# Attention and two mixers on one core: two score products per head from the third tile on, with queries and keys moved by DMAs

## The reference, cut to what matters

```python
# q, k, v: [2, 8, 768, 64] float32; n_sink = 4, window = 128
scores = scale * np.matmul(q, k.transpose(0, 1, 3, 2))
keep = is_sink | in_window            # first 4 keys, and the 128 keys up to the query
scores = np.where(keep, scores, -1e9)
a = softmax(scores)
x = np.matmul(a, v)                   # [2, 768, 512] once the heads are joined
# first mixer:
h = x.transpose(0, 2, 1) @ U @ V      # over tokens, rank 32
u = x + h.transpose(0, 2, 1)
x = u + np.maximum(u @ w_ch1, 0) @ w_ch2
# second mixer: the same with a relu of its own over tokens and other sizes
```

## Time and profile before

| what | us |
|---|---|
| three runs: median (lowest to highest) | 630.93 (630.76 to 631.37) |
| the profiled execution | 631.34 |
| its span, first to last instruction | 629.4 |
| TensorE busy / weight loads busy | 615.7 / 556.5 |
| VectorE, ScalarE, GpSimd busy | 352.6, 324.9, 402.5 |

### The profile page before, as it was taken

How to read it: one execution, slowest core, us unless ns; L and a number is a source line. 1 busy time by engine, 2 the same in 40 slices (tenths; PEclk the granted TensorE clock), 3 DMA queues, 4 the chain that set the end, 5 groups by cost and what they waited for, 6 DMA issues and landing times.

```text
span 629.4 us, 10364 instructions
## 1 busy us (share of the span) xinstructions
PE 615.7 (98%) x3468; PEld 556.5 (88%) x3468; DVE 352.6 (56%) x755; ACT 324.9 (52%) x727; POOL 402.5 (64%) x425
## 2 busy tenths in 40 slices
PE   7899999999999999999999999999999999999997
PEld 6888889999999989999999888899998888999986
DVE  6776664554564646776657731495667227665411
ACT  4666666556545555654544444544453447454321
POOL 7676547978979775665665744567566536666352
PEclk9999999999999999999999999999999999999999
DMA  8482343553343425313223332432324343421152
GB/s 165 94 189 52 84 101 103 134 123 105 96 115 93 151 75 153 100 65 118 85 89 96 111 100 81 128 101 68 117 84 118 112 123 84 150 84 35 51 157 76
DMA packets 88467, 65.59 MB, mean 104 GB/s; under 512 B 43040, under 2 KB 72480, under 8 KB 88416
## 3 DMA queue, kind: packets, MB, share of 16 engines
q1 hardware_dynamic: 88416, 64.95, 37.5%
HBM read 61.52 MB, written 3.15 MB: 103 GB/s over the span
## 4 chain that ended last, share of the span: by engine, by line
PE 87%; DVE 4%; issue 2%; ACT 2%; POOL 2%; DMA 1%; DVEq 0%; SPq 0%; ACTq 0%; POOLq 0%
PE bank L1621 34%; PE bank L1371 23%; PE bank L1586 10%; PE bank L1447 4%; PE bank L1417 3%; PE bank L1550 3%; PE bank L1500 3%; PE bank L1427 2%; PE bank L1526 1%; PE bank L1394 1%; POOL w_lo L879 1%; DVE masked L1142 1%; PE bank L1481 1%; PE bank L1613 1%; ACT probs L898 1%
## 5 line engine op out<-in xcount | busy, mean ns | idle before, releaser
L879 POOL TENSOR_TENSOR w_lo<-w_raw,w_hi 128x512 fp32r<-128x512 f32 (+1 forms) x158 | 210.2, 1337 | 138.3 <-ACT w_hi L912 137.3
L912 ACT ACTIVATE w_hi<-w_raw 128x512 fp32r<-128x512 f32 (+1 forms) x158 | 96.6, 618 | 53.9 <-PE bank L1621 35.9
L1621 PE MATMUL bank<-w_hi,hid_hi 128*128 128x512 f32 x216 | 86.4, 400 | 0.0
L1621 PE MATMUL bank<-w_hi,hid_lo 128*128 128x512 f32 x216 | 85.1, 394 | 0.0
L1621 PE MATMUL bank<-w_lo,hid_hi 128*128 128x512 f32 x216 | 84.8, 393 | 0.0
L898 ACT ACTIVATE probs<-masked,neg_max 128x264 f32<-128x264 f32 x96 | 49.5, 516 | 65.3 <-DVE neg_max L1142 64.8
L1621 PE MATMUL bank<-w_hi,y_hid 128*128 128x512 f32 x216 | 71.1, 394 | 0.2
L1142 DVE CUSTOM_DVE_ANT_0 masked<-bank,masks 128x264 f32<-128x264 f32 x96 | 41.0, 429 | 31.0 <-PE bank L1417 27.6
L1447 PE MATMUL bank<-v_nat,probs_T 128*128 128x64 f32 x352 | 50.2, 261 | 0.8 <-DVE probs_T L1161 0.5
L1447 PEld LDWEIGHTS bank<-v_nat,probs_T 128*128 128x128 f32 x352 | 47.9, 190 | 2.2 <-ACT probs_T L960 0.8
L1621 PEld LDWEIGHTS bank<-w_hi,y_hid 128*128 128x128 f32 x216 | 40.6, 188 | 9.5 <-POOL w_lo L879 1.5
(11 more groups left out here) (177 smaller groups left out, 1501.1 us busy)
## 6 DMA issues: line engine op xcount, KB each, us to landing
w_raw<-in_moe_w_ch_dram SPq DMA_DIRECT2D x144, 256.0 KB, 2.7
w_raw<-in_moe_w_ch_dram SPq DMA_DIRECT2D x20, 512.0 KB, 3.5
q_nat<-in_q_dram SPq DMA_DIRECT2D x12, 256.0 KB, 3.3
k_nat<-in_k_dram SPq DMA_DIRECT2D x12, 256.0 KB, 4.0
v_nat<-in_v_dram SPq DMA_DIRECT2D x12, 256.0 KB, 3.7
out_dram<-o_stage SPq DMA_DIRECT2D x11, 256.0 KB, 3.3
w_raw<-in_moe_w_tok_dram SPq DMA_DIRECT2D x6, 256.0 KB, 2.7
w_raw<-in_moe_w_tok_dram SPq DMA_DIRECT2D x8, 192.0 KB, 2.3
```

What stands on the lines that cost most here:

```text
L879: nc.gpsimd.tensor_tensor(w_lo[:, split % NW, 0:n], w_raw[:, split % NR, 0:n], w_hi[:, split % NW, 0:n].bitcast(f32), ALU.subtract) \
L912: nc.scalar.activation(w_hi[:, split % NW, 0:n], w_raw[:, split % NR, 0:n], ACT.Copy) \
L1621: last = mm(m_tile(use)[:, :], stationary, w[:, slot, :], start=False, stop=(final and n == 2), skip_group_check=True)
```

## The change

The number of the first tile with two products goes from 6 to 2 (`TWO_PASSES_FROM`). For tiles 0 and 1, with three products, the high keys are in an array of their own, `k_one`, which lies where `uT_hi` will be. The copies into the other half are DMAs on SP's queue now, in all tiles from 2 on: two for the queries when `q_hi` is cast, two for the keys when `k_hi` is cast. When tile 1's keys are cast, 12 DMAs bring them and the sinks from `k_one` into `k_hi`, both halves. VectorE's and ScalarE's copies in tiles 6 to 11 are gone, but for the sinks at the second batch's start. TensorE waits at a tile's first score for these DMAs.

```diff
+    TWO_PASSES_FROM = 2
...
+        def high_keys(T):
+            return k_one if T < TWO_PASSES_FROM else k_hi
...
         def query_low(eng, wait, T):
-            if T >= NQ:
+            if T >= TWO_PASSES_FROM:
...
+            def move_queries(T):
+                sp.wait_ge(q_high, T + 1)
+                for e in range(2):
+                    rows, there = slice(e * D, (e + 1) * D), slice((1 - e) * D, (2 - e) * D)
+                    sp.dma_start(q_both[there, T % 2, :, e, :].bitcast(f32), q_hi[rows, T % 2, :, :].bitcast(f32)) \
+                      .then_inc(q_there[T % 2], 16)
+
+            def move_keys(T):
+                sp.wait_ge(k_high, T)
+                for e in range(2):
+                    rows, there = slice(e * D, (e + 1) * D), slice((1 - e) * D, (2 - e) * D)
+                    sp.dma_start(k_hi[there, :, e, T % 3, 0:P].bitcast(f32), k_hi[rows, :, e, T % 3, 0:P].bitcast(f32)) \
+                      .then_inc(k_there[T % 2], 16)
+
+            def move_first_keys(T):
+
+                slot = T % 3
+                sp.wait_ge(k_first_high, 2)
+                sp.wait_ge(k_high, T)
+                for e in range(2):
+                    rows = slice(e * D, (e + 1) * D)
+                    for there in (rows, slice((1 - e) * D, (2 - e) * D)):
+                        sp.dma_start(k_hi[there, :, e, slot, :].bitcast(f32), k_one[rows, :, e, slot, :].bitcast(f32)) \
+                          .then_inc(k_there[slot], 16)
+                        for other in ((slot + 1) % 3, (slot + 2) % 3):
+                            sp.dma_start(k_hi[there, :, e, other, P:BLK].bitcast(f32),
+                                         k_one[rows, :, e, slot, P:BLK].bitcast(f32)).then_inc(ksinks_there, 16)
...
-                elif s[0] == "ksplit" and s[1] >= NQ:
-                    T = s[1]
-                    act.wait_ge(k_copied, T + 1)
-                    act.wait_ge(scores_ready, H * (T - 1))
-                    for e in range(2):
-                        src = list(key_parts(k_hi, T))[e][0]
-                        last = nc.scalar.activation(k_hi[(1 - e) * D:(2 - e) * D, :, e, T % 3, 0:P], src, ACT.Copy)
-                    last.then_inc(k_moved, 1)
...
                     nc.vector.tensor_copy(q_hi[:, T % 2, :, :], q_full).then_inc(q_high, 1)
-                    if T >= NQ:
-                        for e in range(2):
-                            rows, there = slice(e * D, (e + 1) * D), slice((1 - e) * D, (2 - e) * D)
-                            moved = nc.vector.tensor_copy(q_both[there, T % 2, :, e, :], q_full[rows])
-                        moved.then_inc(q_moved, 1)
...
+                        if T == TWO_PASSES_FROM:
+                            pe.wait_ge(k_there[1], 64)
+                            pe.wait_ge(ksinks_there, 128)
+                        if T >= TWO_PASSES_FROM:
+                            pe.wait_ge(q_there[T % 2], 32 * (T // 2))
+                            pe.wait_ge(k_there[T % 2], 32 * (T // 2) + 64 * (T % 2))
...
-                    if T < NQ:
-                        passes = ((high, k_hi), (high, k_lo), (low, k_hi))
+                    if T < TWO_PASSES_FROM:
+                        passes = ((high, k_one), (high, k_lo), (low, k_one))
                     else:
                         passes = ((q_both[:, T % 2, h // 2, h % 2, :], k_hi), (high, k_lo))
```

More of the change, by code:

```diff
@@ L365, in attention_then_two_mixers @@
             k_lo = eb("k_lo", [P, PAIRS, 2, 3, BLK], f32r)
+            with ExitStack() as before_uT:
+                k_one = before_uT.enter_context(nc.sbuf_tensor("k_one", [P, PAIRS, 2, 3, BLK], f32r))
             uT_hi = eb("uT_hi", [P, KD, S], f32r)
@@ L426, in attention_then_two_mixers @@
         klo_zeroed = sem("klo_zeroed")
+        q_there = [sem(f"q_there{i}") for i in range(2)]
+        k_there = [sem(f"k_there{i}") for i in range(2)]
+        ksinks_there = sem("ksinks_there")
         x2_added = sem("x2_added")
@@ L442, in attention_then_two_mixers @@
         q_high = sem("q_high")
-        q_moved = sem("q_moved")
         k_moved = sem("k_moved")
@@ L537, in queries_split @@
         def queries_split(T):
-            return T + 1 if T < NQ else 2 * (T + 1) - NQ
+            return T + 1 if T < TWO_PASSES_FROM else 2 * (T + 1) - TWO_PASSES_FROM
         def query_low(eng, wait, T):
-            if T >= NQ:
+            if T >= TWO_PASSES_FROM:
                 for e in range(2):
@@ L554, in key_low @@
         def key_low(eng, wait, T, e):
-            low, high = list(key_parts(k_lo, T))[e], list(key_parts(k_hi, T))[e]
+            low, high = list(key_parts(k_lo, T))[e], list(key_parts(high_keys(T), T))[e]
             steps = ((3, 2), (1, 0)) if T == 0 else ((1, 0),)
@@ L749, in _ @@
                     loaded = NR
+                elif s[0] == "qsplit" and s[1] >= TWO_PASSES_FROM:
+                    move_queries(s[1])
+                elif s[0] == "ksplit" and s[1] >= TWO_PASSES_FROM - 1:
+                    if s[1] == TWO_PASSES_FROM - 1:
+                        move_first_keys(s[1])
+                    else:
+                        move_keys(s[1])
                 if s in chunk_at:
@@ L917, in _ @@
                     act.wait_ge(q_split, queries_split(T - 1))
-                    if T > NQ:
-                        act.wait_ge(q_moved, T - NQ)
                     act.wait_ge(tp_ready, tp_at[s] + 1)
@@ L934, in _ @@
                     act.wait_ge(k_copied, 1)
-                    for src, dst, sinks, sink_dst in key_parts(k_hi, 0):
+                    for src, dst, sinks, sink_dst in key_parts(k_one, 0):
                         nc.scalar.activation(sink_dst, sinks, ACT.Copy)
                         nc.scalar.activation(dst, src, ACT.Copy).then_inc(k_first_high, 1)
-                elif s[0] == "ksplit" and s[1] >= NQ:
-                    T = s[1]
-                    act.wait_ge(k_copied, T + 1)
-                    act.wait_ge(scores_ready, H * (T - 1))
-                    for e in range(2):
-                        src = list(key_parts(k_hi, T))[e][0]
-                        last = nc.scalar.activation(k_hi[(1 - e) * D:(2 - e) * D, :, e, T % 3, 0:P], src, ACT.Copy)
-                    last.then_inc(k_moved, 1)
                 elif s[0] == "ksinks":
@@ L1062, in _ @@
             for part in (slice(0, 3, 2), slice(1, 2)):
-                nc.vector.memset(k_hi[:, :, :, part, :].rearrange("p a b s k -> p (a b) s k").bitcast(f32), 0.0) \
+                nc.vector.memset(k_one[:, :, :, part, :].rearrange("p a b s k -> p (a b) s k").bitcast(f32), 0.0) \
                   .then_inc(khi_zeroed, 1)
@@ L1118, in _ @@
                         dve.wait_ge(scores_ready, H * (T - 1))
-                    for src, dst, _, _ in key_parts(k_hi, T):
+                    for src, dst, _, _ in key_parts(high_keys(T), T):
                         last = nc.vector.tensor_copy(dst, src)
@@ L1401, in _ @@
                         pe.wait_ge(q_split, queries_split(T))
-                        if T >= NQ:
-                            pe.wait_ge(q_moved, T - NQ + 1)
-                            pe.wait_ge(k_moved, T - NQ + 2)
+                        if T == TWO_PASSES_FROM:
[4 more added lines that the diff above has]
+                            pe.wait_ge(k_there[T % 2], 32 * (T // 2) + 64 * (T % 2))
+                        if T == NQ:
+                            pe.wait_ge(k_moved, 1)
                         pe.wait_ge(k_split, keys_split(T) - (2 if T == 0 else 0 if T == NQ else 1))
```

2 lines of the change are left out of this document (removed).

## The result

The changed kernel takes 640.92 us (median of 4, 639.47 to 641.55) beside 631.11 us of the kernel before (4 runs): ratio 1.0154, 95% interval 1.0142 to 1.0166. The forecast was 632.8 with a range up to 636.0. The sign was right, but the loss is 9.8 us where 1.9 was forecast. The profiled execution took 641.43 us, with a span of 639.7.

What follows compares the result with a forecast made beforehand. VectorE's key casts, held by GpSimd, were taken to bound the first batch, TensorE the stretch from 80 to 200 us. Lost products (3.84 us) go into waiting, held casts net +1.92, moves zero: 632.8 us, range 629.7 to 636.0.

Steps and rivals of the forecast that it cites:

- What bounds: First batch: the end of VectorE's key casts sets each mark; from 80 to 200 us TensorE alone sets the time.
- what a product is worth: Score products of tiles 2 to 5: 0.12 us of TensorE each, 32 lost, 3.84 us.
- The rival with TensorE as the bound: Whole kernel: TensorE sets the end and every lost product shows, 627.1 us; chance 0.14.
- The held casts: Tiles 1 to 4: two GpSimd low-query subtractions (the pair) add 1.40 us and hold VectorE's key casts; sum +1.92 us.
- marks: Starts of line 1481 (x_nat with U) in tiles 1 to 5; forecast at 26.46, 37.38, 49.12, 61.50, 72.19 us.
- Case (b): Tiles 3 and 4: casts ready during the first half-subtraction, one slips in after each half, ending 0.29 us after the pair.
- The rival of casts that stay together: Tiles 3 and 4: both casts run after the first half, 0.93 us earlier in each; 631.0 us; chance 0.24.
- One sign of being right: Marks of tiles 2 to 5: TensorE idles 1.5 us or more before each.
- Hidden, by 0.7 us: Tile 2's first score, wanted at 29.69 us: last key move lands at 29.0, so SP's added moves cost nothing.
- The rival of late moves: Tile 2's last key move lands at 31.7 us, 2.0 late: 634.8 us; later tiles too, 636 and more; chance 0.15.
- the later tiles: First scores after tile 2: key moves land 3.1 us after the casts, wanted 4.39 after; hidden by 1.3 us.

Runs made afterwards that it cites:

- the run with both edits: Kernel before with low queries of tiles 2 to 5 as two GpSimd instructions and their third score product dropped, no DMAs added: 635.64 us, ratio 1.0074.
- the split low queries: Kernel before, three products everywhere, low queries of tiles 2 to 5 made by two GpSimd instructions of 64 partitions: 634.31 us, ratio 1.0060.
- the lost products: Kernel before without the third score product in tiles 2 to 5, nothing else changed: 629.39 us, ratio 0.9976.
- few fills: The run with both edits plus five products of zeros ahead of the marks of tiles 3 and 4: 633.17 us, ratio 1.0038 (1.0025 to 1.0051).
- the one with ScalarE's sinks: Changed kernel with ScalarE copying the sinks in place of eight of the 12 first moves: 637.30 us, ratio 1.0098.
- the odd heads' low queries: Changed kernel with ScalarE copying the sinks and, in tiles 2 to 6, GpSimd's odd-head low queries put behind the first low keys: 631.31 us, ratio 1.0009.

## Why the prediction was wrong

- **What bounds, and what a product is worth: right.** Products of 0.12 us, gone, brought 1.5 of 3.84 us or less. The rival with TensorE as the bound (627.1) is out.
- **The held casts: right, term by term.** The forecast's distances between marks agree to 0.2 us with the run that has this effect alone, and its 632.8, a ratio of 1.0030, lies in that run's interval, 1.0025 to 1.0051. Case (b) was the doubtful one. In tile 3 of the run with both edits the pair ends at 47.56 (44.88 + 2.68) and the casts at 47.85 (45.31 + 2.54), 1.70 us behind the first half, where 1.69 was forecast. The Trainium skill, SBUF — State Buffer, section "Who interferes with whom", read to the letter as first come first served, gave 2.12 behind it. No run here shows that: the first cast's record ends at 46.43, when that of the second half has begun (46.23), so the two overlap. The rival of casts that stay together and end before the second half is out too. One sign of being right did not come, though: of the 1.5 us or more of idle time before each mark, this run shows 1.00, 1.97, 2.13 and 0.70.
- **"Hidden, by 0.7 us": wrong, and the first step that failed.** The second key move should have been issued at 26.6, landed at 29.0 and been wanted at 29.69. It was issued at 27.81, landed at 31.18, released the score at 31.53, and was wanted at 29.03. Each size was a little too favourable. The 12 first moves took until 24.2 in place of 23.5, the first of them 1.15 us to issue. The two query moves took 1.56 in place of 1.3. The landing was put at 2.4 us, from the on-chip copy in the trace before; here the key moves take 3.3 in the median and this one 3.37. And TensorE came 0.66 us sooner, as the start-up was shorter. The rival of late moves had the right place and got 0.15. Its mechanism, a landing of 5.1 us, was half of it: the issue was 1.2 us late and the landing 1.0 longer. So it is partly luck that its 2.0 us of waiting came near the 2.50 measured. For the later tiles the moves landed in time (by 2.9 us in tile 4), but for tile 3: there the last key move took 4.40 us to land, and TensorE waited 0.6.
- **The clock: missing altogether, and the largest term.** The forecast saw that the saved products turn into idle time at the marks, listed "TensorE idles 1.5 us or more" as a sign that it was right, and priced that idle time as nothing. It has no term for the clock, as if the 0.999 of the kernel before were a constant. But in that kernel no idle piece in these tiles is over 0.91 us, and so its trace could not show what a longer one does. Both other terms made such pieces, and 4.4 us of clock came on top. The two terms of the forecast do add up as long as the clock stays: by the ratios the split low queries (+3.8) and the lost products (-1.5) sum to +2.3, and together with few fills they cost 2.4; the four distances between marks add up to 0.1 us each. Without the fills the two cost 4.7. What the sum lacked is the clock's fall, which neither edit alone brought in its profiled execution.
- **The range.** It took in late moves at tile 2, or in all tiles, as one more item beside the sum. What it lacked was a term for what waiting does to the work behind it.

## What to carry to other kernels

Where a change takes work from an engine that waits for another, the saving becomes waiting, and on TensorE longer waiting can cost more than the work did: look at how long each idle piece will be, and not only at their sum. Count the issues of a queue, not their bytes. Eight copies of 4 KB ahead of the moves cost 3.5 us here, the clock's part counted in, and ScalarE made them in four instructions at no cost that shows. And when two engines get in each other's way, look for an instruction that isn't wanted yet and put it behind the other's work, as with the odd heads' low queries, which alone gave back 5.4 of the 9.7 us.

## What the hardware showed that I had not expected

- TensorE's granted clock fell to the 1.2 GHz level in or just behind single idle pieces of 1.88, 2.12, 2.13, 2.14, 2.50 and 4.13 us, in stretches where it was otherwise busy, and stayed there for 3.4 to 6.8 us. But the length of the piece doesn't decide alone: behind 1.97 us (mark 3 of the run with both edits, and of the one with ScalarE's sinks) and 1.92 us (mark 4 of the split low queries alone) it stayed at the 2.4 GHz level, and runs of one kernel differ. The Trainium skill, TensorE: Matmul & The Clock Gate, Part 1, says that the array runs at 1.2 GHz after it was idle and at 2.4 GHz after it was busy; the rows agree with these two levels.
- A few products of zeros inside an idle piece (five at each of two marks, 1.25 us by their rows) made a kernel 2.3 us faster. Twice as many at four marks gave that back.
- Eight of the 12 first moves write pieces of 16 bytes (the sinks' columns). They landed sooner than the moves of 128 KB; no run has a copy of 4 KB in larger pieces beside them, so a penalty for small pieces is neither seen nor ruled out. The DMAs of the changed kernel between 20 and 45 us, by KB each and us to landing:
```profile
q_both<-q_hi SPq DMA_DIRECT2D x4, 128.0 KB, 3.8
k_hi<-k_hi SPq DMA_DIRECT2D x4, 128.0 KB, 3.3
...
k_hi<-k_one SPq DMA_DIRECT2D x4, 4.0 KB, 2.2
```
What they cost is SP's time to issue them, 0.62 us each in most cases.
